# Earlier embeddings, fewer stack copies, spaced gathers, a moved weight request and unread products on TensorE in a fused attention, expert and feed-forward kernel

## The reference

```python
# attention: batch 4, 8 heads, 576 positions, head size 64; rotate() is the rotary embedding
scores = matmul(rotate(q), rotate(k).transpose) / sqrt(64)
x = softmax(scores) @ v                       # then 2304 tokens x 512
# experts, top 1 of 8
logits = (x / norm(x)) @ (expert_emb / norm(expert_emb)).T / tau
x = gate * (relu(x @ w1[e]) @ w2[e])          # e = argmax of the token's logits; w1 512x1024, w2 1024x512
# dense feed-forward
h = x @ w_in                                  # 512 x 2048
out = (h - tanh(h)) @ w_out                   # 2048 x 512
```

## Time and the profile before

| | before |
|---|---|
| time, median of 3 runs | 1083.88 us (1081.81 to 1085.83) |
| profiled execution, its own time | 1088.51 us |
| its span | 1086.7 us |
| mean granted TensorE clock | 0.974 |
| TensorE busy | 988.8 us (91%) |
| VectorE busy | 601.9 us (55%) |
| ScalarE busy | 582.1 us (54%) |
| GpSimd busy | 425.6 us (39%) |
| DMA | 107.98 MB, mean 99 GB/s |

### The profile page before, as it was taken

How to read it: one execution, slowest core, us unless ns; L and a number is a source line. 1 busy time by engine, 2 the same in 40 slices (tenths; PEclk the granted TensorE clock), 3 DMA queues, 4 the chain that set the end, 5 groups by cost and what they waited for, 6 DMA issues and landing times. The chain is left out here.

```text
span 1086.7 us, 18640 instructions
## 1 busy us (share of the span) xinstructions
PE 988.8 (91%) x5624; PEld 877.4 (81%) x5625; DVE 601.9 (55%) x1198; ACT 582.1 (54%) x1276; POOL 425.6 (39%) x226
## 2 busy tenths in 40 slices
PE   2699999999998299999999947999999999999996
PEld 2699989899897278888888746889989889888895
DVE  4677777777776641111111115776666666666664
ACT  2477777777776542222222225656565565665553
POOL 2987878878710189169957041000000000000000
PEclk9999999999999599999999978999999999999999
DMA  8666656566742574124431053210000000000001
GB/s 240 182 188 163 172 171 179 168 174 161 259 113 68 197 251 146 59 80 146 146 106 58 21 157 86 59 49 30 1 29 0 0 29 0 29 0 0 30 1 30
DMA packets 58225, 107.98 MB, mean 99 GB/s; under 512 B 19264, under 2 KB 24896, under 8 KB 55872
## 3 DMA queue, kind: packets, MB, share of 16 engines
q1 hardware_dynamic: 50576, 89.62, 28.1%
q0 software_dynamic: 3440, 11.27, 3.3%
q10 hardware_dynamic: 4160, 6.44, 1.7%
HBM read 61.89 MB, written 17.03 MB: 73 GB/s over the span
## 5 line engine op out<-in xcount | busy, mean ns | idle before, releaser
L1612 PE MATMUL hd_ps<-y_hi,w_hi 128*128 128x384 f32 x384 | 132.4, 345 | 10.9 <-DVE g_sb L1781 6.3
L1681 ACT ACTIVATE mag<-hd_ps 128x384 f32<-128x384 f32 x96 | 47.3, 493 | 158.1 <-PE hd_ps L1612 154.2
L1612 PE MATMUL hd_ps<-y_hi,w_lo 128*128 128x384 f32 x384 | 130.9, 341 | 0.0
L1612 PE MATMUL hd_ps<-y_lo,w_hi 128*128 128x384 f32 x384 | 130.7, 340 | 0.0
L1009 DVE TENSOR_TENSOR pt_lo<-ps,pt_hi 128x512 fp32r<-128x512 f32 x144 | 99.1, 689 | 44.1 <-ACT pt_hi L767 42.6
L993 DVE TENSOR_REDUCE neg_max<-ps 128x1 f32<-128x576 f32 x144 | 107.9, 750 | 26.8 <-PE ps L575 24.2
L1790 DVE TENSOR_TENSOR g_lo<-g_sb,g_hi 128x384 fp32r<-128x384 f32 x96 | 53.5, 558 | 117.5 <-ACT g_hi L1696 117.5
L1630 PE MATMUL o_ps<-w_hi,g_hi 128*128 128x512 f32 x288 | 115.5, 401 | 3.3 <-DVE g_lo L1790 2.2
L767 ACT ACTIVATE pt_hi<-ps 128x512 fp32r<-128x512 f32 x144 | 86.9, 605 | 58.8 <-PE ps L622 57.5
L1630 PE MATMUL o_ps<-w_lo,g_hi 128*128 128x512 f32 x288 | 114.7, 398 | 0.0
L1630 PE MATMUL o_ps<-w_hi,g_lo 128*128 128x512 f32 x288 | 114.1, 396 | 0.0
(11 more groups left out here) (226 smaller groups left out, 2427.7 us busy)
## 6 DMA issues: line engine op xcount, KB each, us to landing
raw_qk<-in_qk SPq DMA_DIRECT2D x14, 1152.0 KB, 5.4
w_stage<-in_w SPq DMA_DIRECT2D x28, 512.0 KB, 3.6
k_hh<-qk_hi SPq DMA_DIRECT2D x64, 144.0 KB, 2.6
k_ll<-qk_lo SPq DMA_DIRECT2D x64, 144.0 KB, 2.8
y_rows<-y_row ACTq DMA_DIRECT2D x20, 256.0 KB, 2.0
q_st<-qk_hi SPq DMA_DIRECT2D x30, 144.0 KB, 3.0
q_st<-qk_lo SPq DMA_DIRECT2D x30, 144.0 KB, 2.9
raw_v<-in_v SPq DMA_DIRECT2D x32, 128.0 KB, 2.2
```

The source lines that it names most:

```text
L1612: op = nc.tensor.matmul(hd_ps[f % 2][:, 0:G], w[:, c, cols], y[:, c, :], start=c == 0 and h == 0, stop=c == DC - 1 and h == 2)
L1681: nc.scalar.activation(mag[r][:], hd_ps[r][:, 0:G], ACT.Abs).then_inc(mag_done, 1)
```

## The change

It has seven parts.

1. Embeddings and newton: ScalarE requests the embeddings ahead of the tables. VectorE squares them before it rotates k, clamps the norms behind that, and makes `newton` and the division by tau behind q's rotation, ahead of pair 1's two products. ScalarE takes the root ahead of its four q copies. The two scalings of `fold_sb` go from VectorE to GpSimd, behind `add_up(1, ...)`, and wait for `emb_scale`.
2. Copies: `k_hh` and `k_ll` stand in one tensor, `hi` and `lo` in another, so that one copy moves both parts of k: `stack_k` issues 4 instead of 8, a pair 8 instead of 12.
3. Unread products: `keep_running(n)` issues n products of the `zeros` tile (128 x 128 by 128 x 256) into a part of PSUM that nobody reads: 18 behind the root of the embeddings' norms and ahead of the first scores, 24 behind `ranked`, 16 behind `ids_ready`. The experts' block has 20 unread transposes between `turn_x(0)` and `up_first`.
4. The w2 request of the first expert moves from the end of attention to SyncE's first place in the experts' block.
5. Experts' gathers: `AHEAD` is 5. Tiles 1 to 4 are gathered at the opening; the others wait for the first set's split and go two ahead of each chunk of the second set's split (`two_more`).
6. Dense gathers: each of the 13 waits until step f of the first group has used its operands (`g_used`).
7. `zeros` is of the matmul's type, and `tile_eq` has another address.

```diff
-AHEAD = HELD - 8
+AHEAD = 5
...
-        STACKS = 12 * 16
+        STACKS = 8 * 16
...
-        k_hh = [[put(f"k_hh{r}{u}", [P, S], F32R) for u in range(2)] for r in range(2)]
-        k_ll = [[put(f"k_ll{r}{u}", [P, S], F32R) for u in range(2)] for r in range(2)]
+        k_st = [[put(f"k_st{r}{u}", [P, 2, S], F32R) for u in range(2)] for r in range(2)]
+        k_hh, k_ll = ([[k_st[r][u][:, part, :] for u in range(2)] for r in range(2)] for part in range(2))
...
-        hi = put("qk_hi", [P, 2, S], F32R)
-        lo = put("qk_lo", [P, 2, S], F32R)
+        qk_split = put("qk_split", [P, 2, 2, S], F32R)
+        hi, lo = (qk_split[:, part, :, :] for part in range(2))
...
-        zeros = put("zeros", [P, D])
+        zeros = put("zeros", [P, D], F32R)
...
-        tile_eq = spots(nc, lo_at)("tile_eq", [P, T, MT])
+        tile_eq = spots(nc, w_at + 3 * SET // 4)("tile_eq", [P, T, MT])
...
             def stack_k(r, landed=None):
...
-                    rows = slice(u * DH, (u + 1) * DH)
+                    both = qk_split[u * DH:(u + 1) * DH, :, 1, :].bitcast(F32)
                     for half in range(2):
-                        to = slice(half * DH, (half + 1) * DH)
-                        sp.dma_start(k_hh[r][u][to, :].bitcast(F32),
-                                     hi[rows, 1, :].bitcast(F32)).then_inc(landed[u], 16)
-                        sp.dma_start(k_ll[r][u][to, :].bitcast(F32),
-                                     lo[rows, 1, :].bitcast(F32)).then_inc(landed[u], 16)
+                        sp.dma_start(k_st[r][u][half * DH:(half + 1) * DH, :, :].bitcast(F32), both).then_inc(landed[u], 16)
             def stack_q(r):
-                for half, part in enumerate((hi, lo)):
-                    to = slice(half * DH, (half + 1) * DH)
-                    for u in range(2):
-                        sp.dma_start(q_st[r][u][to, u * TAIL:u * TAIL + S].bitcast(F32),
-                                     part[u * DH:(u + 1) * DH, 0, :].bitcast(F32)).then_inc(stack_in[r], 16)
+                for u in range(2):
+                    for half in range(2):
+                        sp.dma_start(q_st[r][u][half * DH:(half + 1) * DH, u * TAIL:u * TAIL + S].bitcast(F32),
+                                     qk_split[u * DH:(u + 1) * DH, half, 0, :].bitcast(F32)).then_inc(stack_in[r], 16)
...
             sp.wait_ge(x_stored, 16 * 2 * (B + 1))
-            sp.wait_ge(sq_done, T)
-            for c in range(UP, CHUNKS):
-                sp.dma_start(early_half(rows, c), weight_chunk(a["w1"], a["w2"], expert, c)).then_inc(second_half[c - UP], 16)
...
             add_up(1, 0, 1, first=True)
+            pool.wait_ge(consts_in, 16 * 6)
+            pool.wait_ge(emb_scale, 1)
+            by_emb = emb_n[:, 4, :].unsqueeze(1).to_broadcast([P, PB, E])
+            nc.gpsimd.tensor_tensor(fold_sb[:, :, 0:E], fold_sb[:, :, 0:E], by_emb, ALU.mult)
+            nc.gpsimd.tensor_tensor(fold_sb[:, :, FW:FP], fold_sb[:, :, FW:FP], by_emb, ALU.mult).then_inc(fold_scaled, 1)
...
+            def keep_running(times):
+                for _ in range(times):
+                    nc.tensor.matmul(ps[:, 3584:3840], zeros[:, 0:P], zeros[:, 0:2 * P], start=True, stop=True)
+            pe.wait_ge(zero_set, 2)
+            pe.wait_ge(emb_root, 1)
+            keep_running(18)
             pe.wait_ge(cleared, 1)
             for i in range(TILES):
                 scores(0, 0, i, 0, first=True)
...
                              stop=True).then_inc(ranked, 1)
+            keep_running(24)
...
             last.then_inc(ids_ready, 1)
+            keep_running(16)
...
+            act.dma_start(emb_sb[:], a["emb_t"].rearrange("(c p) e -> p c e", p=P)).then_inc(emb_in, 16)
             act.dma_start(cos_sb[:, 1, :], a["cos"]).then_inc(tables_in, 16)
             act.dma_start(sin_sb[:, 1, :], a["sin"]).then_inc(tables_in, 16)
-            act.dma_start(emb_sb[:], a["emb_t"].rearrange("(c p) e -> p c e", p=P)).then_inc(emb_in, 16)
...
+            act.wait_ge(emb_clamped, 1)
+            nc.scalar.activation(emb_n[:, 1, :], emb_n[:, 0, :], ACT.Sqrt).then_inc(emb_root, 1)
             act.wait_ge(cleared, 1)
             act.wait_ge(rope_done, 1)
             for u in range(2):
-                for half, part in enumerate((hi, lo)):
-                    to = slice(half * DH, (half + 1) * DH)
-                    act.dma_start(q_st[0][u][to, u * TAIL:u * TAIL + S].bitcast(F32),
-                                  part[u * DH:(u + 1) * DH, 0, :].bitcast(F32)).then_inc((first_a, stack_in[0])[u], 16)
-            act.wait_ge(emb_clamped, 1)
-            nc.scalar.activation(emb_n[:, 1, :], emb_n[:, 0, :], ACT.Sqrt).then_inc(emb_root, 1)
...
+            dve.wait_ge(emb_in, 16)
+            nc.vector.tensor_tensor(emb_sq[:], emb_sb[:], emb_sb[:], ALU.mult).then_inc(emb_squared, 1)
             dve.wait_ge(tables_in, 32)
             rope_first(1, first_k_in, first_k_mult, first_k_done)
-            dve.wait_ge(emb_in, 16)
-            nc.vector.tensor_tensor(emb_sq[:], emb_sb[:], emb_sb[:], ALU.mult).then_inc(emb_squared, 1)
+            dve.wait_ge(emb_summed, 1)
+            nc.vector.tensor_scalar(emb_n[:, 0, :], norm_ps, 1e-30, None, ALU.max).then_inc(emb_clamped, 1)
             dve.wait_ge(table_scaled, 2)
             rope_first(0, first_q_in, mult_done, rope_done)
-            dve.wait_ge(emb_summed, 1)
-            nc.vector.tensor_scalar(emb_n[:, 0, :], norm_ps, 1e-30, None, ALU.max).then_inc(emb_clamped, 1)
+            dve.wait_ge(tau_in, 16)
+            chain(nc.vector.reciprocal(inv_tau, tau_sb))
+            dve.wait_ge(emb_root, 1)
+            newton(chain, nc, emb_n[:, 2, :], emb_n[:, 1, :], emb_n[:, 0, :], emb_n[:, 3, :])
+            nc.vector.tensor_scalar(emb_n[:, 4, :], emb_n[:, 2, :], inv_tau, None, ALU.mult).then_inc(emb_scale, 1)
             dve.wait_ge(second_in, 16)
             nc.vector.tensor_tensor(by_cos[:], raw1[:, 0:2, :], cos_sb[:], ALU.mult)
             nc.vector.tensor_tensor(by_sin[:], raw1[:, 2:4, :], sin_sb[:], ALU.mult).then_inc(mult_done, 1)
             for i in range(TILES):
                 maximum(0, 0, i)
-                if i == MIX:
-                    dve.wait_ge(tau_in, 16)
-                    chain(nc.vector.reciprocal(inv_tau, tau_sb))
-                    dve.wait_ge(emb_root, 1)
-                    newton(chain, nc, emb_n[:, 2, :], emb_n[:, 1, :], emb_n[:, 0, :], emb_n[:, 3, :])
-                    chain(nc.vector.tensor_scalar(emb_n[:, 4, :], emb_n[:, 2, :], inv_tau, None, ALU.mult))
-            dve.wait_ge(consts_in, 16 * 6)
-            by_emb = emb_n[:, 4, :].unsqueeze(1).to_broadcast([P, PB, E])
-            nc.vector.tensor_tensor(fold_sb[:, :, 0:E], fold_sb[:, :, 0:E], by_emb, ALU.mult)
-            nc.vector.tensor_tensor(fold_sb[:, :, FW:FP], fold_sb[:, :, FW:FP], by_emb, ALU.mult).then_inc(fold_scaled, 1)
             body(0, 0, first=True)
...
         def _(sp):
+            expert = sp.value_load(plan[0:1, FIRST, 0:1], min_val=0, max_val=E - 1)
+            for c in range(UP, CHUNKS):
+                sp.dma_start(early_half(rows, c), weight_chunk(w1, w2, expert, c)).then_inc(second_half[c - UP], 16)
...
-            def split_set(before, slot):
+            def split_set(before, slot, between=None):
                 for c in range(CHUNKS):
+                    if between:
+                        between(c)
...
+            def two_more(c):
+                for t in range(AHEAD + 2 * c, min(AHEAD + 2 * c + 2, HELD)):
+                    gather(t)
             pool.wait_ge(one_set, 1)
             pool.wait_ge(w_split, CHUNKS)
             last = pool.value_load(plan[0:1, LAST, 0:1], min_val=0, max_val=E - 1)
-            for t in range(AHEAD, HELD):
+            with pool.If(last > 0):
+                slot = pool.value_load(plan[0:1, SLOT, 1:2], min_val=0, max_val=1)
+                split_set(0, slot, two_more)
+            with pool.If(last < 1):
+                for t in range(AHEAD, HELD):
+                    gather(t)
+            for t in range(AHEAD + 2 * CHUNKS, HELD):
                 gather(t)
-            with pool.Fori(0, 3) as before:
+            with pool.Fori(1, 3) as before:
                 next_set(before)
...
             turn_x(0)
+            for _ in range(20):
+                nc.tensor.transpose(y_ps[:, 0:P], id_sb[:], id_sb[:])
             up_first()
...
             for f in range(KF):
                 if GT + f < T - 2:
+                    pool.wait_ge(g_used, f + 1)
                     gather(GT + f)
```

More of the change, by code:

```diff
@@ L146, in attention @@
         pt_lo = put("pt_lo", [P, FULL + 1, MAIN], F32R)
-        lo_at = w_at + 4 * (10 * S + 4 * WIDE + (FULL + 1) * WIDE_PT)
         v_split1 = put("v_split1", [P, TILES + 2, 2 * DH], F32R)
@@ L280, in attention @@
         emb_root = sem("emb_root")
+        emb_scale = sem("emb_scale")
         fold_scaled = sem("fold_scaled")
@@ L444, in _ @@
             for t in range(T, MT):
```

(23 more changed lines are left out.)

## The result

The changed kernel takes 1072.97 us (median of 4 runs, 1072.59 to 1073.30), the kernel before 1083.52 beside it (4 runs, 1081.81 to 1085.83). The ratio is 0.9901, 95% interval 0.9882 to 0.9920: faster by 10.6 us, where 15.8 were forecast (1068.1, range 1062.5 to 1077.5). A second set on one chip gives 1072.39 (5 runs) against 1083.02 (14 runs), ratio 0.9906 (0.9892 to 0.9920). Two further runs of the kernel before, 1118.8 and 1259.0 us at a granted clock of 0.88 and 0.74, are slow ones and left out of every number here.

A forecast was written before the change was run, and what follows sets the result against it. TensorE is busy nearly throughout, so gains must come from idle time in three stretches: opening, routing, dense opening. -7.3 - 0.4 - 0.4 - 0.7 - 7.0 = -15.8 from 1083.9 gives 1068.1 us, range 1062.5 to 1077.5.

The forecast's parts named there:

- rival 2: Opening: packets take turns from the start, tables land at 10.6, opening gains only 3.0, total 1072.4 us; chance 0.12.
- Opening, -7.3: Start to first pair body: tables at 7.0, newton moved, fewer copies; body starts at 36.1 instead of 43.4 us.
- Index products, -0.4: Routing, 24 unread products: if the clock stays up, index products end sooner after VectorE; -0.4 us (0 to -1.4).
- Opening stretch, 0: 18 unread products ahead of the first scores: shorten only scores that the stack chain covers; 0.
- Fourth stretch, -0.4: Experts' opening, 20 unread transposes: clock rises during them for the first opening products; -0.4 us (+1.4 to -1.7).
- w2, 0: Moved w2 request at the experts' start: gather freed, but block waits for VectorE; 0, up to +2 if cover fails.
- Experts, -0.7: Experts' block: spacing the gathers removes the late signal that cost TensorE 0.73 us; -0.7 us (0 to -1).
- Dense, -7.0: Dense opening: spaced gathers end late signals, first output product at 656.0 instead of 661.90; -7.0 us (0 to -7.7).
- Rival 1: Experts' and dense blocks: late signals are not the gathers', so 7.7 us are not gained, 1075.8 us; chance 0.22.
- Rival 3: Dense opening: each of 13 spaced gathers holds a signal, net +26.3, 1110.2 us; chance 0.05.
- Rival 4: Clock stays up throughout: 2.0 at the body, 1.0 index products, 1.3 fourth stretch more, 1063.8 us; chance 0.08.
- the copies' bounds (8.0 and 10.9): Opening, pair 1's stack copies, taken as 9.0 us: low bound from 8 issues and last landing, high the old time.

The follow-up runs named there:

- twelve-copies run: Changed kernel with k's two parts copied one by one, 12 copies a pair instead of 8, same memory layout: 1071.80 us (5 runs).
- prompt: Outcome of the kernel before with no late signals in the dense opening: 1081 to 1086 us in two sets; the late outcome is mostly 1087 to 1093.
- the spaced runs: Kernel before with only its 13 dense gathers spaced: 1083.15 us (6 runs), against a median of 1090.3 beside it without spacing.
- the request through GpSimd: Changed kernel with the embeddings requested by GpSimd instead of ScalarE, so the tables are first on ScalarE's queue: 1071.05 us (6 runs).

## Why the prediction was right, and where it was not

The time lies in the range, 4.9 us above the point, and 0.6 above rival 2's 1072.4, whose condition (tables at 10.6) was not met. The direction and most of the mechanisms were right, the size was so in part by luck. By its steps:

- **Opening, -7.3: mis-sized.** The chain was right: tables, rotations, pair 1's sums, copies, body. "I take 7.0" for the tables should have been 8.57 (1.6 us, half way to rival 2's 10.6), and "9.0 us" for the copies was 10.1 from 28.81 to 38.89; in between VectorE needed 0.6 less than forecast and GpSimd 0.8 more, most of it a wait for q's copies. "8 issues instead of 12 save about 2.5 us of queue" is refuted by the twelve-copies run. On the other side the old opening is not a fixed 43.4 either: it is 44.49 in the trace of the kernel before with w2 moved and 45.94 in the one with spaced gathers, where VectorE's two `fold_sb` steps took up to 2.03 and 1.39 us while GpSimd worked. And one bound was summed wrongly: tables 3.6 us later than 7.0 leave -3.7, not -3.0, so rival 2 should have read 1071.7.
- **Index products, -0.4: right** (4.04 to 3.63; with the same 24 products ahead of them they took 2.98 to 4.04 in other traces). **Opening stretch, 0: right.**
- **Fourth stretch, -0.4: mis-sized.** 1.9 in the profiled pair, just beyond its range (+1.4 to -1.7), and 0.8 in the second profile of the changed kernel (10.0 against 10.8 us).
- **w2, 0: wrong.** "The block waits for VectorE anyway" overlooked that the block also waits for GpSimd's gather. The rows had it: 2.4 us between VectorE's end and the block's opening, noted and not asked after. It is -1.9 in the traces and -1.1 in the times of the kernel before.
- **Experts, -0.7:** the profiled pair shows it, because its execution of before had the late signal; the prompt executions have nothing to gain there. From the end of the opening products to the dense block's first turn it is 257.9 us in that execution, 257.2 in the changed kernel and 257.2 in the prompt kernel before with w2 moved.
- **Dense, -7.0: right mechanism, wrong as a constant.** The profiled execution had a stall that the three timed runs shown did not have. "It lies 4.6 above the median; the same difference gives 1068.1" is the step that failed: the 4.6 were that stall, so a gain that consists of removing it could not be carried over to the median. Read so, 7.0 + 0.7 should have come off 1088.5 only, which leaves 1075.8 for the median, and w2's 1.9 makes it 1073.9. Rival 1 gave 1075.8 on the ground that the signals are not the gathers'; the spaced runs refute the ground, as far as more than the spacing itself is meant: why a signal is late stays open.
- **Rival 3**, a late signal at each spaced gather: absent. **Rival 4**, the clock up throughout: 0.83 and 0.79 in the windows, so no.

The reading behind the copies' bounds (8.0 and 10.9) was wrong. `qk_hi` at 40.42 does not show when the copies had landed, because GpSimd was busy until then:

```profile
37.83 2.67 POOL L515 TENSOR_TENSOR rotated<-by_cos,by_sin 128x1152 f32<-128x1152 f32 x1
```

The last copy was issued at 36.5 and took 2.9 us to landing, so all had landed by 39.5, 9.9 us behind the sum: twelve copies had taken no longer than the eight do. With that row read, the copies would have stood at 9.9 and not at 9.0.

Of the -2.4 us behind the first output product some 1.7 are another thing: at the change from the first group to the second TensorE idles 1.9 us in the kernel before and 1.5 in the changed one, and only in the former the clock falls for 3.4 us after it (0.95 against 1.00):

```profile
700.00:735.00 35.00, 32.55 (x158) 28.33 (x157) 25.12 (x54) 20.65 (x46) 2.00 (x2) 0.95 0.17 51
```

```profile
690.00:720.00 30.00, 28.18 (x142) 24.12 (x141) 21.81 (x46) 18.84 (x42) 5.78 (x6) 1.00 0.31 85
```

All three traces of the kernel before and of kernels made from it have this drop, with spaced gathers too (idle for 1.87 to 1.89 us), and none of the eleven of the changed kernel and of those made from it (1.51 to 1.53). No edit touches the code of this place, and why the idle time differs stays open. Nor do the listed parts add up to the medians' 10.6 exactly: opening 4.5 to 7, w2 1.1 to 1.9, unread work (index products included) 1.7, the drop 1.7, less 1.0 for the dense opening (13.9 against 12.9 us, at a lower clock) is 8.0 to 11.3. The opening's part is read from traces; no run took its edits apart, other than the copies. That time saved there comes off the whole is shown by the request through GpSimd: the body 1.6 us sooner, the kernel 1.7 faster.

## What to carry to other kernels

Ask whether the profiled execution is one of those that the median describes: if its own time lies outside the range of the timed runs, find which stall makes it so before pricing the removal of that stall. At a boundary where all engines meet, look for a transfer under way beside the last busy engine, for what is late there may be a DMA that another DMA holds up. And the number of copies is no price where their bytes fill the DMA engines, as they did here.

## What the runs showed of the hardware

- A finished product's signal reached ScalarE up to 6.4 us after its last product (652.01 and 658.40 in the kernel before) instead of 0.04 (642.95 and 642.99 in the changed kernel), during or up to 2.6 us after a run of indirect gathers that GpSimd issued one behind the other (1.25 us apart), in some sets of runs in nearly every run and in others in none, with the same program. No trace with one gather a step (4.2 to 4.7 us) showed it.
- All engines left a block only when GpSimd's gather had landed, and 2 MB of loads issued ahead of it raised its time to landing from 3.8 to 6.0 us.
- Eight SBUF-to-SBUF copies, four of them twice as large, took 7.6 us to issue, as did twelve: 0.92 and 0.97 us each against 0.62, with the DMA engines 92 to 94% busy in both.
- VectorE's smallest steps are not constant: `fold_sb`'s scaling of 32 columns took 0.69, 2.03 and 2.03 us in three traces while GpSimd was at work, and 0.25 on GpSimd itself. `newton`'s steps on 128x8 took 0.17 to 0.20 each with GpSimd idle and up to 2.57 beside its sums.
- Unread work keeps TensorE's clock: 70 transposes in a 12.4 us hole lifted the granted clock from 0.74 to 0.90 between the block's first turn and 652, for 1.7 us by the medians.
